# Attention, mixture of experts and FFN on one core: another order of VectorE's work in the paired Strassen steps

## The reference

```python
# attention: softmax over 31 neighbours and 24 block maxima, times v
p = domain_probs / (domain_probs.sum(-1, keepdims=True) + 1e-09)
for e in range(4):                           # x 1536x512, w1 512x1024, w2 1024x512
    h = np.maximum(x @ w1[e], 0.0)
    out += p[:, e:e + 1] * (h @ w2[e])
h = out @ w_in                               # 512x2048
g = h * (1.0 / (1.0 + np.exp(-1.702 * h)))
y = g @ w_out                                # 2048x512
```

## Time and profile before

| | |
|---|---|
| median of three runs | 829.47 us |
| profiled execution | 831.31 us, span 829.3 us |
| TensorE matmul busy | 798.4 us, 96% |
| VectorE busy | 598.7 us, 72% |
| GpSimd busy | 582.1 us, 70% |
| ScalarE busy | 399.2 us, 48% |
| TensorE's granted clock, mean | 0.996 of full speed |

### The profile page before, as it was taken

How to read it: one execution, slowest core, us unless ns; L and a number is a source line. 1 busy time by engine, 2 the same in 40 slices (tenths; PEclk the granted TensorE clock), 3 DMA queues, 4 the chain that set the end, 5 groups by cost and what they waited for, 6 DMA issues and landing times.

```text
span 829.3 us, 13946 instructions
## 1 busy us (share of the span) xinstructions
PE 798.4 (96%) x4894; PEld 780.4 (94%) x4894; DVE 598.7 (72%) x1194; ACT 399.2 (48%) x863; POOL 582.1 (70%) x406
## 2 busy tenths in 40 slices
PE   4889999999999999999999999999999999999997
PEld 3778999999999999999999999999999999999997
DVE  5878666666665566798888888665665665789787
ACT  3765445444444454435344344434555553555552
POOL 3596665565666699678788684777488783688784
PEclk9989999999999999999999999999999999999999
DMA  9958558375444354446245343343544544363412
GB/s 259 274 134 287 235 181 271 140 243 203 183 158 193 140 205 161 175 149 237 99 192 187 130 189 141 139 191 140 223 160 176 193 166 188 144 251 140 177 53 76
DMA packets 39956, 148.91 MB, mean 180 GB/s; under 512 B 16208, under 2 KB 17360, under 8 KB 36688
## 3 DMA queue, kind: packets, MB, share of 16 engines
q1 hardware_dynamic: 39888, 148.03, 49.5%
HBM read 100.81 MB, written 47.21 MB: 178 GB/s over the span
## 4 chain that ended last, share of the span: by engine, by line
PE 81%; DVE 8%; issue 4%; ACT 3%; POOL 3%; DMA 1%; SPq 0%; DVEq 0%; ACTq 0%; POOLq 0%
PE bank L1615 26%; PE bank L1617 26%; PE bank L1616 26%; DVE xa L1333 2%; ACT prob L938 1%; PE bank L1570 1%; DVE xb_last_lo L1339 1%; PE bank L1607 1%; DMA v_cols<-v_t 1%; PE bank L1581 1%; DVE h_raw L1384 1%; DVE xb_first_lo L1339 1%; POOL wu_lo L719 1%; POOL wd_lo L731 1%; DVE masked L1253 0%
## 5 line engine op out<-in xcount | busy, mean ns | idle before, releaser
L1321 DVE TENSOR_TENSOR xa<-bank,xa 128x384 f32<-128x384 f32 x208 | 115.7, 556 | 136.1 <-PE bank L1617 133.2
L1615 PE MATMUL bank<-h_hi,wd_hi 128*128 128x384 f32 x448 | 150.5, 336 | 0.2 <-DVE xa L1319 0.2
L1617 PE MATMUL bank<-h_lo,wd_hi 128*128 128x384 f32 x448 | 149.8, 334 | 0.0
L1616 PE MATMUL bank<-h_hi,wd_lo 128*128 128x384 f32 x448 | 149.7, 334 | 0.0
L731 POOL TENSOR_TENSOR wd_lo<-stage,wd_hi 128x1024 fp32r<-128x1024 f32 x27 | 65.2, 2415 | 86.4 <-ACT wd_hi L986 86.3
L1029 ACT ACTIVATE h_hi<-bank 128x384 fp32r<-128x384 f32 x112 | 55.1, 492 | 138.1 <-DVE bank L1379 114.8
L1013 ACT ACTIVATE snap<-bank 128x384 f32<-128x384 f32 x141 | 69.2, 490 | 102.6 <-PE bank L1617 101.8
L798 POOL TENSOR_TENSOR wd_lo<-stage,wd_hi 128x512 fp32r<-128x512 f32 x60 | 82.7, 1385 | 50.3 <-ACT wd_hi L1061 50.3
L1615 PE MATMUL bank<-xb_other_hi,wu_hi 128*128 128x384 f32 x336 | 112.4, 335 | 0.2 <-ACT snap L1013 0.2
L1617 PE MATMUL bank<-xb_other_lo,wu_hi 128*128 128x384 f32 x336 | 112.3, 334 | 0.0
L1616 PE MATMUL bank<-xb_other_hi,wu_lo 128*128 128x384 f32 x336 | 112.2, 334 | 0.0
(11 more groups left out here) (121 smaller groups left out, 2101.9 us busy)
## 6 DMA issues: line engine op xcount, KB each, us to landing
stage<-weights SPq DMA_DIRECT2D x25, 1024.0 KB, 4.9
split<-wu_hi SPq DMA_DIRECT2D x24, 896.0 KB, 3.6
split<-wu_lo SPq DMA_DIRECT2D x24, 896.0 KB, 5.4
wu_hi<-split SPq DMA_DIRECT2D x23, 896.0 KB, 6.0
wu_lo<-split SPq DMA_DIRECT2D x23, 896.0 KB, 7.7
stage<-weights SPq DMA_DIRECT2D x23, 512.0 KB, 4.5
k_win<-k_w SPq DMA_DIRECT2D x8, 720.0 KB, 8.5
v_win<-v_w SPq DMA_DIRECT2D x8, 576.0 KB, 9.2
```

What stands on the lines that cost most here:

```text
L1321: nc.vector.tensor_tensor(at, y_bank(g, t), at, ALU.add).then_inc(y_taken, 1)
L1615: nc.tensor.matmul(dst, w_h, a_h, start=first, stop=False, skip_group_check=True)
L1616: nc.tensor.matmul(dst, w_l, a_h, start=False, stop=False, skip_group_check=True)
L1617: return nc.tensor.matmul(dst, w_h, a_l, start=False, stop=last, skip_group_check=True)
```

## The change

VectorE's list is reordered in the second step of a pair, in the step after it and in the tail. VectorE's own wait ahead of the taking of P6, for the taking of P3 (both add into the same part of `xa`), is taken out; TensorE's P6 waits for the taking of P3 instead of that of P1. ScalarE splits the weights of P1 (high_held) later in the even step.

```diff
--- before.py
+++ after.py
@@ -1175,8 +1175,6 @@
                     high_moved(ph, 1)
                 if part == 4:
                     high_moved(ph, 6)
-                if paired(g):
-                    high_held(g, "P1")
                 keep(g, 2)
                 for u in turned(g):
                     value_means(u)
@@ -1188,6 +1186,7 @@
                     sigmoid(g, "C21")
                 if paired(g):
                     high_tile(g, "C21")
+                    high_held(g, "P1")
                     high_held(g, "P5")
                 else:
                     high_hidden(g, "C21")
@@ -1323,8 +1322,6 @@
             def take_product(g, name, d):
 
                 dve.wait_ge(y_done, taken(g, name, d))
-                if name == "P6":
-                    dve.wait_ge(y_taken, taken(g, "P3", d))
                 i, c, first = ADDED[name]
                 at, source = xa[1][:, 2 * i + d, tokens(c)], pair_bank(g, name, d)
                 if first and g in FIRST:
@@ -1446,18 +1443,19 @@
                     low_moved(5)
                     take_y(0, 3)
                 elif second(g):
-                    if paired(g - 3):
-                        take_product(g - 3, "P4", 1)
                     if g + 1 < STEPS:
                         take_product(g - 1, "P1", 0)
                     add_c11(g)
                     gate(g, "C11")
                     low_sum(g - 1, 1)
+                    take_product(g - 1, "P1", 1 if g + 1 < STEPS else 0)
                     low_tile(g, "C11")
-                    take_product(g - 1, "P1", 1 if g + 1 < STEPS else 0)
                     add_c22(g)
+                    if g + 1 < STEPS:
+                        take_product(g - 1, "P5", 0)
+                    else:
+                        take_product(g - 1, "P1", 1)
                     gate(g, "C22")
-                    take_product(g - 1, "P5" if g + 1 < STEPS else "P1", 0 if g + 1 < STEPS else 1)
                     gate(g, "C21")
                     add_c12(g)
                     low_tile(g, "C21")
@@ -1465,41 +1463,40 @@
                     low_tile(g, "C22")
                     if g + 1 == STEPS:
                         take_product(g - 1, "P5", 0)
+                    take_product(g - 1, "P5", 1)
                     continue
                 elif paired(g - 1):
-                    take_product(g - 2, "P5", 1)
                     low_tile(g - 1, "C12")
                     take_product(g - 2, "P2", 0)
                     add_c11(g)
                     gate(g, "C11")
+                    low_sum(g - 2, 2)
                     take_product(g - 2, "P2", 1)
-                    low_sum(g - 2, 2)
                     take_product(g - 2, "P3", 0)
+                    low_sum(g - 2, 3)
                     if paired(g):
                         low_tile(g, "C11")
                     else:
                         low_hidden(g, "C11")
-                    low_sum(g - 2, 3)
                     take_product(g - 2, "P3", 1)
                     take_product(g - 2, "P6", 0)
                     add_c22(g)
+                    gate(g, "C22")
+                    low_sum(g - 2, 4)
                     take_product(g - 2, "P6", 1)
-                    gate(g, "C22")
                     take_product(g - 2, "P7", 0)
-                    low_sum(g - 2, 4)
-                    gate(g, "C21")
                     if not paired(g):
                         low_hidden(g, "C22")
+                    gate(g, "C21")
                     take_product(g - 2, "P7", 1)
                     if paired(g):
                         low_tile(g, "C21")
                     else:
                         low_hidden(g, "C21")
                     add_c12(g)
+                    take_product(g - 2, "P4", 0)
                     gate(g, "C12")
-                    take_product(g - 2, "P4", 0)
-                    if not paired(g):
-                        take_product(g - 2, "P4", 1)
+                    take_product(g - 2, "P4", 1)
                     continue
                 else:
                     take_y(g - 1, 0)
@@ -1535,18 +1532,15 @@
                     value_sums(u)
                 for u in unit_after(g, 1):
                     key_maxima(u)
-            take_product(STEPS - 2, "P5", 1)
             low_tile(STEPS - 1, "C12")
             take_product(STEPS - 2, "P2", 0)
+            low_sum(STEPS - 2, 2)
             take_product(STEPS - 2, "P2", 1)
-            low_sum(STEPS - 2, 2)
+            low_sum(STEPS - 2, 3)
             take_product(STEPS - 2, "P3", 0)
             take_product(STEPS - 2, "P3", 1)
-            low_sum(STEPS - 2, 3)
-            take_product(STEPS - 2, "P6", 0)
-            take_product(STEPS - 2, "P6", 1)
             low_sum(STEPS - 2, 4)
-            for name, d in TAKES[IN_PAIR + 6:]:
+            for name, d in TAKES[IN_PAIR + 4:]:
                 take_product(STEPS - 2, name, d)
 
         @block.tensor
@@ -1712,7 +1706,7 @@
                     if d and g + 2 < STEPS:
                         pe.wait_ge(y_taken, taken(g, "P2", 0))
                 else:
-                    pe.wait_ge(y_taken, taken(g, {"P3": "P5", "P6": "P1", "P7": "P6", "P4": "P7"}[name], d))
+                    pe.wait_ge(y_taken, taken(g, {"P3": "P5", "P6": "P3", "P7": "P6", "P4": "P7"}[name], d))
                 hi, lo = moved_2(MOVED[name])
                 w_hi, w_lo = held_2(name)
                 for f in range(2):
```

## The result

The changed kernel takes 838.40 us (median of 4 runs, 837.14 to 840.51) against 829.12 us: ratio 1.011, interval 1.0082 to 1.0139, slower by 9.3 us; 837.3 (+7.8 on a median of 829.47 for the kernel before) was predicted. The profiled execution has a span of 835.4 us. That is only 6.1 us more than before, because its attention part happened to be shorter (untouched, it ends between 339.5 and 344.6 us in the traces of this case), so I compare stages of the traces. They are cut at the first matmul of the first MoE pair product, at the first plain down product behind step 28, at the first FFN pair product, and at the last matmul.

What follows compares the result with a forecast made beforehand. TensorE, 96% busy at full clock, was taken as the bound, so only its standing still counts. 3.45 + 0.35 + 2.85 - 0.25 + 1.4 = 7.8 us on the 829.47 median gave 837.3 us, range 832.5 to 841.0.

Steps and rivals of the forecast that it cites:

- The nine waits before P2 stay: Step after a pair: TensorE's nine waits before P2's second half, together 8.5 us, stay near 0.57 and 0.87 shown.
- P6's second half, 0.57 in 8 steps: Step after a pair: P6's second half starts late behind take(P3,1), 0.57 us in each MoE (18 to 26) and FFN step.
- P7's second half: Step after a pair: it waits for take(P6,1) behind low_sum(4), 0.12 us in MoE steps, 0.35 in step 28, 0.38 in FFN.
- The tail, +1.4: After the last step P6 waits for take(P3,0) behind low_sum(3); last take 1.4 us later, bounds +0.2 and +2.3.
- high_held(P1) costs nothing: ScalarE's later split of P1's weights pushes sum_hidden(1) back some 0.4 us, which low_sum(1) hides: no cost.
- The dropped wait of VectorE is worth nothing: Removing VectorE's wait of P6 behind P3 gives back nothing measurable; both takes already ran 0.47 us apart.
- A: Rival, cheap turns: VectorE and GpSimd meet at luckier phases, P6's second half is on time; +5.0, 834.4 us; chance 0.18.
- C: Rival, no change: P6's wait for take(P3) is always met and low_sum(4) finishes early; under 2 us, 830.5 us; chance 0.07.
- D: Rival, faster: the GpSimd turn behind the P2 wait goes, and the nine waits with it; -8.5 us, 821.0 us; chance 0.06.
- B: Rival, drift: GpSimd's chain half a microsecond late delays second steps by 0.5 in 9 pairs; 841.8 us; chance 0.09.
- Some 27: Sign: TensorE's waits on line 1333, the taking of a product, should rise from 10 to some 27.
- The turns: VectorE's two-SBUF-input subtractions and GpSimd instructions alternate, blocking each other; one blocked turn fewer makes the sum about 7, not 7.8.

Runs made afterwards that it cites:

- sliver run: Changed kernel with GpSimd's four weight sums of a pair cut to 16 of 256 columns, so the output differs; 836.15 us, ratio 1.0078.
- wait alone: Kernel before with one edit: TensorE's P6 waits for the take of P3 instead of that of P1; 833.02 us, ratio 1.0049.
- old waits: Changed kernel with TensorE's P6 waiting for P1's take again and VectorE's wait ahead of P6's take restored, new order kept; 836.70 us, ratio 1.0089.
- filler run: Changed kernel with 15 more matmuls, result unused, behind P3's second half in the tail; 837.21 us, ratio 1.0081.
- P6 early: Changed kernel with take(P6,1) ahead of gate(C22) and low_sum(4) again in the step after a pair; 835.91 us, ratio 1.0087.
- held early: Changed kernel with ScalarE's high_held(P1) back at its old place, ahead of keep(g, 2); 840.47 us, ratio 1.0141.

## Why the prediction was right, and where not

The direction and the size were right: +9.3 us measured, +9.5 in the two changed stages of the traces, +7.8 forecast. The 1.7 us that the forecast lacks against the stages are 1.5 us of clock in the tail, for which it had no term, and small misses of both signs that nearly cancel. By its own steps:

- *The nine waits before P2 stay.* They did: 0.56 shown in the six MoE pairs, 0.87, 0.84 and 0.84 in the FFN pairs. The first FFN pair, forecast 0.25 better, came out 0.32 better (1.19 to 0.87).
- *P6's second half, 0.57 in 8 steps.* Measured 0.56. It takes both the turns (they are gone in the sliver run, and P6 waits nowhere) and TensorE's new wait, which costs the same in the old order (wait alone).
- *P7's second half.* 0.38 in the FFN steps against 0.39 measured, 0.35 in step 28 against 0.37; 0.12 in the MoE steps was undersized, 0.20. Together with P6's it is the stage's +4.26 (5 x 0.77 + 0.38 = 4.23). The two aren't independent costs: take out P6's wait and P7's grows by as much (old waits), since P7 is held by gate(C22) and low_sum(4), which stay where they are.
- *The tail, +1.4.* The wait was placed rightly. The order itself added 2.1 us from P3 on (11.81 less 9.70, the filler run), and P3 came 0.44 us earlier (its wait fell from 0.72 to 0.28), together +1.7, so the term was 0.3 too small. The term left out is the clock: 1.5 us. These pieces with the FFN steps' 2.85 and the shorter P2 waits (0.39) make 5.6, some 0.4 more than the stage moved. Matmul by matmul the two traces show where that lies: at 742.03, 772.40, 810.00 and 813.23 us the kernel before has restarts 0.07 to 0.11 us long (a bar of 0.41 or 0.44 for 0.33, with no idle time shown) that the changed kernel has not.
- *high_held(P1) costs nothing.* This step failed. It is worth 3.1 us: without it low_held(P1) falls on low_sum(4) in the FFN steps. The forecast sum came out right because I laid out the new GpSimd order without that instruction there, but I booked the move at zero and did not see that it was a part that wins. That much of the agreement was luck: the prediction works out where the instruction goes, but nowhere what it did at its old place.
- *The dropped wait of VectorE is worth nothing.* No run took it away alone. With both waits back (the run of both old waits), the steps after a pair cost the same.
- *Rivals.* A, C and D are out. B (drift by GpSimd's chain) did not appear: the second steps show no new wait.
- *The signs.* "Some 27" waits was a miscount: the prediction's own steps list 9 before P2, 8 before P6, 3 before P7 and one in the tail, 21, and 21 were measured. Low_tile(C11) ended after line 788, as said, but did not begin before it (391.10 against 390.44).
- *The turns.* The forecast's "about 7" for one turn fewer has no sum behind it; the sliver run, where GpSimd's sums hardly block, is 2.2 us below the changed kernel. The rule on a VectorE instruction with two SBUF inputs, which the prediction cites, stands in the Trainium skill's page SBUF — State Buffer under "Who interferes with whom", not in the section that it names. This case agrees: line 1336 took 1.64 us beside the full sums and 0.61 beside the slivers.

## What to carry to other kernels

On an in-order engine a finished result is handed on only when the instructions ahead are done: put the short instruction that frees a bank ahead of a long one that may have to wait for its turn, and measure each order in the one wait that it is meant for. A wait removed where the next one hangs on the same chain gives nothing; moved instructions of a third engine may be what keeps two others apart. And count an idle TensorE twice: once for the wait, and again if the clock falls behind it.

## What the runs showed of the hardware that I had not expected

Behind 3.17 to 3.20 us of idle TensorE in the tail the granted clock fell to the 1.2 GHz level in all four profiled runs that had it (changed kernel, P6 early, sliver, held early), and 9 to 11 matmuls ran at it, which cost 1.4 to 1.6 us; behind 2.49 us (old waits) and 0.64 (filler) it did not. It fell with the first matmul behind the wait in the sliver and P6-early runs, some 1.2 us later in the held-early run and 1.8 us later in the changed kernel. The Trainium skill, TensorE: Matmul & The Clock Gate, section "Part 1: The HAM clock gate (the "warmup" mystery)", gives exactly these two levels; the trace agrees, 0.32 us from matmul to matmul at the lower and 0.17 at the upper.
